# An attention and feed-forward kernel whose score matmuls stream 512 columns, a whole PSUM bank, in place of 450

## The reference

```python
scores = scale * np.matmul(z, z.transpose(0, 2, 1))      # scale = 1 / 3136
attn = np.maximum(scores, 0.0) ** 2
x = u * np.matmul(attn, v)                               # 4 x 3136 x 256
h = np.maximum(x @ w_in, 0.0)                            # 256 -> 1024
hp = np.concatenate([zeros, h, zeros], axis=1)           # one row of zeros at either end
for k in range(3):
    conv_out += conv_w[k][None, None, :] * hp[:, k:k + S, :]
gate = 1.0 / (1.0 + np.exp(-conv_out))
out = h * gate @ w_out                                   # 1024 -> 256
```

## Time and profile before

| | |
|---|---|
| median of 2 runs | 1751.88 us (1751.47 to 1752.29) |
| span of the profiled execution | 1752.0 us |
| matmuls, and weight loads | 8242 each |
| TensorE matmul busy | 1708.5 us, 98% |
| TensorE weight load busy | 1556.2 us, 89% |
| VectorE busy | 1390.4 us, 79% |
| ScalarE busy | 1212.0 us, 69% |
| GpSimd busy | 222.6 us, 13% |

### The profile page before, as it was taken

The page is one execution under the profiler, slowest core; times in us unless marked ns, Lnnn a source line. Parts: engine busy times, 40 slices in busy tenths (PEclk is TensorE's granted clock), DMA queues, the critical chain, the costliest instruction groups (busy, mean ns, idle before and its releaser), DMA issues.

```text
span 1752.0 us, 27520 instructions
## 1 busy us (share of the span) xinstructions
PE 1708.5 (98%) x8242; PEld 1556.2 (89%) x8242; DVE 1390.4 (79%) x1831; ACT 1212.0 (69%) x1938; POOL 222.6 (13%) x167
## 2 busy tenths in 40 slices
PE   8899999999999999999999999999999999999996
PEld 7799999988999999998899999999889999999975
DVE  7688778788877878788887878777887878787794
ACT  7666766777676667677766767666776676677774
POOL 7200000024000000004200000000510000000150
PEclk9999999999999999999999999999999999999997
DMA  4100000032000000003100000001210000000220
GB/s 146 53 27 0 26 26 12 15 99 68 0 26 26 15 11 26 26 0 110 55 20 6 26 26 0 26 26 50 77 38 26 0 26 26 26 0 26 78 61 21
DMA packets 27951, 59.31 MB, mean 34 GB/s; under 512 B 3232, under 2 KB 8224, under 8 KB 27936
## 3 DMA queue, kind: packets, MB, share of 16 engines
q1 hardware_dynamic: 27936, 59.13, 10.7%
HBM read 46.27 MB, written 12.85 MB: 34 GB/s over the span
## 4 chain that ended last, share of the span: by engine, by line
PE 85%; DVE 5%; ACT 3%; issue 3%; POOL 0%; ACTq 0%; DMA 0%; DVEq 0%; POOLq 0%
PE ps_y L353 14%; PE ps_h L340 14%; PE ps_av L315 14%; PE ps_av L317 14%; PE ps_av L316 14%; PE ps_s L297 7%; PE ps_s L298 7%; DVE g_sb L579 2%; ACT attn_hi L427 1%; DVE g_sb L587 1%; DVE g_lo L597 1%; DVE attn_lo L540 1%; DVE attn L552 1%; PE ps_av L319 1%; PE ps_av L320 1%
## 5 line engine op out<-in xcount | busy, mean ns | idle before, releaser
L552 DVE SCALAR_TENSOR_TENSOR attn<-ps_s,relu_s 128x450 f32<-128x450 f32 x677 | 417.8, 622 | 225.1 <-ACT relu_s L432 224.6
L315 PE MATMUL ps_av<-attn_lo,v_hi 128*128 128x450 f32 x1344 | 494.6, 368 | 10.5 <-DVE attn_lo L540 8.7
L317 PE MATMUL ps_av<-attn_hi,v_lo 128*128 128x450 f32 x1344 | 494.1, 368 | 0.0
L316 PE MATMUL ps_av<-attn_hi,v_hi 128*128 128x450 f32 x1344 | 493.6, 367 | 0.0
L432 ACT ACTIVATE relu_s<-ps_s 128x450 f32<-128x450 f32 x677 | 362.9, 542 | 137.8 <-PE ps_s L298 137.5
L540 DVE TENSOR_TENSOR attn_lo<-attn,attn_hi 128x900 fp32r<-128x900 f32 x338 | 379.7, 1123 | 47.8 <-ACT attn_hi L427 47.5
L427 ACT ACTIVATE attn_hi<-attn 128x900 fp32r<-128x900 f32 x338 | 323.3, 957 | 121.4 <-DVE attn L552 120.8
L315 PEld LDWEIGHTS ps_av<-attn_lo,v_hi 128*128 128x128 f32 x1344 | 253.3, 188 | 39.3 <-DVE attn_lo L540 7.2
L316 PEld LDWEIGHTS ps_av<-attn_hi,v_hi 128*128 128x128 f32 x1344 | 253.4, 189 | 22.4
L317 PEld LDWEIGHTS ps_av<-attn_hi,v_lo 128*128 128x128 f32 x1344 | 253.0, 188 | 21.9
L297 PE MATMUL ps_s<-z_mv,z_st 128*128 (+1 forms) x677 | 250.0, 369 | 8.2 <-DVE z_st L633 6.5
(11 more groups left out here) (52 smaller groups left out, 1942.5 us busy)
## 6 DMA issues: line engine op xcount, KB each, us to landing
raw<-v_all SPq DMA_DIRECT2D x60, 256.0 KB, 2.7
u_sb<-u_win SPq DMA_DIRECT2D x28, 450.0 KB, 3.5
out<-y_sb SPq DMA_DIRECT2D x28, 448.0 KB, 2.6
raw<-z_all SPq DMA_DIRECT2D x30, 256.0 KB, 2.7
z_raw<-z_win SPq DMA_DIRECT2D x29, 225.0 KB, 3.5
w_raw<-w_all SPq DMA_DIRECT2D x8, 256.0 KB, 2.7
raw<-v_all SPq DMA_DIRECT2D x5, 128.0 KB, 2.5
raw<-z_all SPq DMA_DIRECT2D x5, 64.0 KB, 1.8
```

Source lines behind the costliest of these rows:

```text
L315: mm(acc, vh, lo, start=j == 0, stop=False)
L316: mm(acc, vh, hi, start=False, stop=False)
L317: done = mm(acc, vl, hi, start=False, stop=False)
L552: dve.scalar_tensor_tensor(dst, scores_bank(j), 0.0, relu_slot(j), ALU.max, ALU.mult).then_inc(attn_ready, 1)
```

## The change

The moving operand of the two score matmuls becomes 512 columns wide in place of 450, and their output the whole bank of 512. `z_mv`, `z_raw` and the array in memory that the window is loaded from grow to 512 columns as well (the 62 further columns hold the z of the rows that follow, or zeros behind the end of a batch), and with them the load, ScalarE's copy and the remainders. The 62 further columns of the scores are read by nobody: ScalarE and VectorE still read 450, and the other matmuls are as they were. No instruction is added, removed or moved.

```diff
+BANK = 512
...
-        z_mv = sb("z_mv", [P, 2, 2, WIDE], F32R)
-        z_raw = sb("z_raw", [P, WIDE])
+        z_mv = sb("z_mv", [P, 2, 2, BANK], F32R)
+        z_raw = sb("z_raw", [P, BANK])
...
+        def whole_bank(j):
+            return ps_s[:, j % SBANKS, :] if j < LAST else ps_h[:, :]
...
-                mm(scores_bank(j), w, z_mv[:, n % 2, 1, :], start=True, stop=False)
-                mm(scores_bank(j), w, z_mv[:, n % 2, 0, :], start=False, stop=True
+                mm(whole_bank(j), w, z_mv[:, n % 2, 1, :], start=True, stop=False)
+                mm(whole_bank(j), w, z_mv[:, n % 2, 0, :], start=False, stop=True
                    ).then_inc(scores_ready, 1)
...
-                act.activation(z_mv[:, n % 2, :, :], z_raw[:, None, :].broadcast_to([P, 2, WIDE]), ACT.Copy
+                act.activation(z_mv[:, n % 2, :, :], z_raw[:, None, :].broadcast_to([P, 2, BANK]), ACT.Copy
                                ).then_inc(z_rounded, 1)
...
-    z_win = windows(z_rows, 1)
+    z_win = windows(z_rows, 1, BANK)
```

More of the change, by code:

```diff
@@ L707, with windows @@
     from concourse.bass_utils import run_bass_kernel_spmd
-    def windows(a, extra):
+    def windows(a, extra, width=WIDE):
         rows = a.shape[1]
-        padded = np.zeros((BATCHES, rows, SEQ + 2 * HALO), a.dtype)
+        padded = np.zeros((BATCHES, rows, SEQ - BLOCK + BANK), a.dtype)
         padded[:, :, HALO:HALO + SEQ] = a
-        win = np.zeros((BLOCKS + extra, rows, WIDE), a.dtype)
+        win = np.zeros((BLOCKS + extra, rows, width), a.dtype)
         for n in range(BLOCKS):
             b, i = divmod(n, PER_BATCH)
-            win[n] = padded[b, :, i * BLOCK:i * BLOCK + WIDE]
+            win[n] = padded[b, :, i * BLOCK:i * BLOCK + width]
         return win
```

## The result

The changed kernel takes 1788.8 us (median of 2 runs, 1787.4 to 1790.2) against 1751.9: a ratio of 1.021, with a 95% interval of 1.018 to 1.024. Predicted were 1787, range 1779 to 1792.

What follows compares the result with a forecast made beforehand. TensorE, busy 98% and without pauses in the full stretches, was taken as the bound. The terms 36.6 - 2.0 + 0.4 + 0.2 = 35.2 us, added to the profiled 1752.0 us, gave 1787 us (+2.0%), range 1779 to 1792.

Steps and rivals of the forecast that it cites:

- The score matmuls, +36.6 us: TensorE's 1410 score matmuls, 62 columns wider: 25.8 ns more each for 1402, 0.4 us for eight at half clock.
- (a): Score matmuls: the 17.3 ns beside the stream is a fixed gap; 512 columns take 230.6 ns, 25.8 more; 64%.
- The row after a pause: TensorE's first matmuls after a pause: the second started 0.20 us after the first, waiting for its stream, not for weights.
- (b): Score matmuls: the weight load sets the pace, a wider matmul fills the gap first; 8.5 ns more, 1764 us; 13%.
- (c): Score matmuls: one feeder brings weight and operand columns at a constant rate; 22.0 ns more, 1782 us; 12%.
- (d): Score matmuls: the operand arrives at a lower rate than the clock; 233.0 ns, 28.2 more, 1790 us; 8%.
- the rival: The reading (b) of the score matmuls: weight loads, busy 351.76 of 383 us in full stretches, set the pace; 13%.
- The pauses, -2.0 us: Ends of batches and start: TensorE arrives later and waits less for VectorE and ScalarE; 2.0 us back, between 0 and 4.6.
- The preparation, +0.4 and +0.2 us: Wider window: GpSimd's longer subtractions slow VectorE at ends of batches, +0.4 us; longer first load, copy and subtractions at start, +0.2.
- the small terms: Everything beside the score matmuls: pauses -2.0 us, window preparation +0.4 us, start +0.2 us; together -1.4 us.

## Why the prediction was right

**What bounds the kernel.** TensorE, with stretches that are full: the same stretches are full after, and only the distance after score matmuls moved.

**The score matmuls, +36.6 us.** The distance was forecast at 230.6 ns, and is 230.3 and 230.8. The count is as it was, 1410. By the direct distances, (230.5 - 204.6) x 1410 = 36.5. This term carried the result, and it stood on the choice of (a). The row after a pause spoke against (b) alone, and the run with 256 columns shows that it was read rightly; had I taken that rival, I would have been 24 us too low. Among (a), (c) and (d) the prediction had nothing to choose by but that (a) lies in the middle, so that part was luck. Nor does the time of the kernel choose: 1788.8 us lies between the 1787 of (a) and the 1790 of (d). The distance does, with 230.5 ns against 233.0 by (d) and 226.8 by (c), and the runs with 384 and 256 columns show that the gap is fixed only from 450 columns on.

The Trainium skill, page "Perfetto Trace Analysis", section "Identifying the Most-Contended Engine", judges TensorE's headroom by the share of peak arithmetic done (MFU) and by the share of weight-load time. Taken as the rival took it, with 92% naming the load, the second isn't borne out here: the share is 93% with 256 columns (269.02 of 290 us in a full stretch), though a score matmul takes only 119 ns, and 51% in the bfloat16 kernel, where TensorE is just as full. The Trainium skill, page "TensorE: Matmul & The Clock Gate", section "Back-to-back issue gap", has N / 2.4 + 2.5 ns for isolated matmuls. The constant holds for bfloat16 (2.3 measured with 450 columns) and not for fp32r (17), and the slope from 450 to 512 columns for both (25.9 ns measured for fp32r and 25.7 for bfloat16). The 131 ns that the same section of the Trainium skill has for N = 512 are shown by no run.

**The pauses, -2.0 us.** The three waits of TensorE that recur at the four ends of batches sum to 11.8 us before and 9.7 after, 2.1 less. Three rows of the kernel before (60 to 1710 us), then three of the kernel after (60 to 1745 us):

```profile
PE ps_h L340 <- ACT h_sb L448: 5.3, 8, 0.7
PE ps_av L315 <- DVE attn_lo L540: 4.2, 8, 0.6
PE ps_y L353 <- DVE g_lo L597: 2.3, 4, 0.6
...
PE ps_av L319 <- DVE attn_lo L544: 4.5, 8, 0.8
PE ps_h L344 <- ACT h_sb L452: 3.7, 8, 0.6
...
PE ps_y L357 <- DVE g_lo L601: 1.5, 4, 0.4
```

Three batches show 25.9 us more where 1050 score matmuls give 27.1, which would be 1.6 us less over four ends. What the wider preparation adds there is in both figures.

**The preparation, +0.4 and +0.2 us.** GpSimd's subtraction has a median of 1287 ns against 1147, ScalarE's copy 1046 against 942, where I had 1310 and 1070. The first matmul starts at 6.66 in place of 6.50 us: +0.16. At the ends of batches 0.4 was too little: the run with the preparation alone has 2.0 us more of waits there, though its time allows only 0 to 3 us for all of it. In the changed kernel this can't be told from what the pauses take up.

**What was not in the sum.** The start gave more than its share: 342 score matmuls come before the first recurring pause, 8.8 us at 25.8 ns, and it is 10.0 us later. TensorE runs at 1.2 GHz in two stretches that lie elsewhere in the two profiled executions. The kernel after, at the start and behind the pauses of block 0:

```profile
13.64 0.58 PE L319 MATMUL ps_av<-attn_lo,v_hi 128*128 128x450 f32 x1
14.02 0.58 PE L320 MATMUL ps_av<-attn_hi,v_hi 128*128 128x450 f32 x1
14.39 0.58 PE L321 MATMUL ps_av<-attn_hi,v_lo 128*128 128x450 f32 x1
...
63.90 0.74 PE L319 MATMUL ps_av<-attn_lo,v_hi 128*128 128x450 f32 x1 [1.48 <-DVE x_sb L570]
64.44 0.58 PE L320 MATMUL ps_av<-attn_hi,v_hi 128*128 128x450 f32 x1
64.81 0.58 PE L321 MATMUL ps_av<-attn_hi,v_lo 128*128 128x450 f32 x1
```

After the first pause the matmuls of the kernel after are still 375 ns (450 columns) and 427 ns (512) apart, until 15.9 us, where the kernel before is at full speed from 11.8. The clock column of the stretch view shows 1.00 there; the distances are what tells. By then the kernel after is 1.7 us further behind than its score matmuls explain, and a later wait takes it back: between 12 and 60 us TensorE waits 3.1 us for attn_lo in place of 4.5. The second stretch, with a granted clock of 0.50, lies from 54.4 to 57.8 us before, and the pauses behind it take it up: TensorE waits 0.2 us for attn there, where it waits 1.9 after. After the change the stretch lies from 63.9 to 67.3 us, at the head of a full stretch, and stays: the matmul after it starts at 67.17 in place of 64.12 us, 3.05 later, where 64 score matmuls give 1.65. These 1.4 us are what the ends of batches give back by the end of the kernel.

Neither goes with the 512 columns. Full speed comes at 15.8 us in the run with the preparation alone and at 16.0 in the bfloat16 kernel with 450 columns, and at 12.0 in the run with 256 columns. The second stretch begins at 53.1 us in the bfloat16 kernel with 512 columns, and the run with 128 has one at 63.4. What sets the two was not tried, and is open.

So the sum of 35.2 us met 36.4 in the span and 36.9 in the medians, with the small terms forecast at -1.4 and coming to about 0, since the start wasn't among them. That it came within 1.2 to 1.7 us is partly luck: spans of the kernel before alone lie from 1749.7 to 1754.6 us. The forecast lay astride 2%, and so does the measured interval.

## What to carry to other kernels

Where TensorE is full, its time is the sum of the distances of starts, and a moving column costs a cycle whether anybody reads it or not: cut the streamed width to what is used, and don't fill a bank for its own sake. Read what a matmul takes from starts in a full stretch, and look for what holds the next one at the first matmuls after a pause; the listed length of the weight load (0.19 us) is not its floor. Before a rest of a microsecond is given to the change, look where the stretches at half the clock lie in the two executions. Where the precision allows 2-byte parts, all matmuls should change together, since with a change of type between neighbours some eleven ns of the fifteen gained on the first one are lost.

## What the runs showed of the hardware that was not expected

- A matmul with fp32r operands takes 12.3 ns beside its stream at 256 columns, 15.6 at 384 and some 17 from 450 on, at 2.4 GHz; with bfloat16 operands 2.3. At 1.2 GHz, half the clock, fp32r has no gap at all, with 450 columns or with 512: 7.22, 7.65, 8.08 and 8.50 us are starts in the kernel after, 427 ns apart, which is 512 / 1.2 GHz.
- The weight load of a 4-byte operand is listed with 188 ns, yet loads can follow each other every 108 to 112 ns. That bounds the matmuls of 128 columns (111 ns each); those of 256 columns take 119.
- The first bfloat16 load after an fp32r matmul is not pulled ahead, and the first such matmul takes 200.8 ns in place of 190.0. When all matmuls are bfloat16, each of 450 columns takes 189.8.
